# Feed-forward stage: the last block holds the last 384 tokens in their own order, and its output is stored by plain DMAs

## What is computed

```python
# q, k, v: (4, 8, 576, 64)
out_up    = repeat4(softmax(pool4(q) @ pool4(k).T / 8) @ pool4(v))
out_local = softmax(mask(|i-j| < 4, q @ k.T / 8)) @ v
x = (out_up + out_local).transpose(0, 2, 1, 3).reshape(2304, 512)
# experts: 8, each token goes to one
expert = argmax(normalise(x) @ normalise(emb).T / tau)
gate   = softmax(...)[expert]
x2[expert == e] = gate * (relu(x[expert == e] @ w1[e]) @ w2[e])   # 512 -> 1024 -> 512
# feed-forward: 512 -> 2048 -> 512
h   = x2 @ w_in
out = maximum(0.01 * h, h) @ w_out
```

## Time and profile before

| | us |
|---|---|
| median of 3 runs (lowest, highest) | 929.17 (929.08, 933.5) |
| profiled execution | 922.41 |
| its span | 920.6 |
| TensorE busy in the span | 873.1 (95%) |
| VectorE busy | 537.6 (58%) |
| ScalarE busy | 508.8 (55%) |
| GpSimd busy | 184.0 (20%) |

### The profile page before, as it was taken

The page is one execution under the profiler, slowest core; times in us unless marked ns, Lnnn a source line. Parts: engine busy times, 40 slices in busy tenths (PEclk is TensorE's granted clock), DMA queues, the critical chain, the costliest instruction groups (busy, mean ns, idle before and its releaser), DMA issues.

```text
span 920.6 us, 17203 instructions
## 1 busy us (share of the span) xinstructions
PE 873.1 (95%) x5878; PEld 733.8 (80%) x5878; DVE 537.6 (58%) x789; ACT 508.8 (55%) x912; POOL 184.0 (20%) x265
## 2 busy tenths in 40 slices
PE   8898997899999999999998999999999999999993
PEld 4787773677787777777777998998998998998992
DVE  5677766788888988888886543223223223223221
ACT  3677875788887888888885443223223223223221
POOL 8666773042510110120001002002002002001001
PEclk9999999999999999999999999999999999999997
DMA  7587567354727725541101002002002002000000
GB/s 221 163 236 205 182 223 256 111 192 131 289 53 278 275 94 238 224 144 47 35 23 46 1 1 69 1 1 69 0 0 68 0 0 68 0 0 35 1 1 34
DMA packets 44764, 92.39 MB, mean 100 GB/s; under 512 B 4712, under 2 KB 24040, under 8 KB 40624
## 3 DMA queue, kind: packets, MB, share of 16 engines
q1 hardware_dynamic: 34496, 43.48, 15.7%
q0 software_dynamic: 10224, 48.33, 14.1%
HBM read 72.98 MB, written 18.81 MB: 100 GB/s over the span
## 4 chain that ended last, share of the span: by engine, by line
PE 79%; DVE 6%; ACT 5%; issue 4%; POOL 2%; DMA 1%; SPq 1%; DVEq 0%; ACTq 0%; POOLq 0%
PE banks L857 68%; PE banks L795 2%; PE banks L889 2%; ACT ehi L1107 1%; PE banks L773 1%; PE banks L700 1%; DVE elo L1438 1%; DVE xTlo L1443 1%; PE banks L737 1%; PE banks L749 1%; PE banks L908 1%; PE banks L708 1%; PE banks L864 1%; PE banks L767 1%; ACT pdin L1010 1%
## 5 line engine op out<-in xcount | busy, mean ns | idle before, releaser
L1438 DVE TENSOR_TENSOR elo<-wslot,ehi 128x1024 fp32r<-128x1024 f32 x196 | 237.6, 1224 | 37.9 <-ACT ehi L1107 28.9
L1107 ACT ACTIVATE ehi<-wslot 128x1024 fp32r x196 | 204.9, 1059 | 45.4 <-PE banks L857 36.0
L1512 DVE SCALAR_TENSOR_TENSOR fg<-fraw 128x384 f32<-128x384 f32 x96 | 53.5, 558 | 212.3 <-ACT fraw L1194 212.3
L1194 ACT ACTIVATE fraw<-banks 128x384 f32<-128x384 f32 x96 | 47.2, 492 | 227.8 <-PE banks L857 227.5
L857 PE MATMUL banks<-zhi,winhi 128*128 (+1 forms) x384 | 130.5, 340 | 0.2 <-issue 0.2
L857 PE MATMUL banks<-zhi,winlo 128*128 (+1 forms) x384 | 129.4, 337 | 0.0
L857 PE MATMUL banks<-zlo,winhi 128*128 (+1 forms) x384 | 129.0, 336 | 0.0
L857 PE MATMUL banks<-wouthi,fhi 128*128 128x512 f32 x288 | 113.1, 393 | 3.5 <-DVE flo L1517 3.4
L857 PE MATMUL banks<-wouthi,flo 128*128 128x512 f32 x288 | 113.9, 395 | 0.0
L857 PE MATMUL banks<-woutlo,fhi 128*128 128x512 f32 x288 | 113.7, 395 | 0.0
L656 POOL DMA_INDIRECT out_x<-o_sb,row_tok x18 | 17.9, 995 | 386.0 <-ACT o_sb L1221 382.4
(11 more groups left out here) (206 smaller groups left out, 1432.2 us busy)
## 6 DMA issues: line engine op xcount, KB each, us to landing
wslot<-in_w POOLq DMA_DIRECT2D x24, 1024.0 KB, 9.4
wslot<-in_w SPq DMA_DIRECT2D x8, 1024.0 KB, 6.1
xr<-xs SPq DMA_DIRECT2D x25, 272.0 KB, 2.9
ys<-y_sb SPq DMA_DIRECT2D x25, 256.0 KB, 2.0
qb<-in_qT SPq DMA_DIRECT2D x16, 288.0 KB, 4.0
kb<-in_kT SPq DMA_DIRECT2D x16, 288.0 KB, 5.0
vq<-in_vtok SPq DMA_DIRECT2D x32, 144.0 KB
vwin<-in_vtok SPq DMA_DIRECT2D x16, 245.0 KB
```

The lines of the kernel that those rows point to most:

```text
L1107: act.activation(ehi[:, ring_at(k), :], wslot[:, chunk_cols(offs[dt], matrix, half, c)], ACT.Copy).then_inc(s_ehi, 1)
L1194: act.activation(fraw[:, f % 2, :], banks[:, f % 2, 0:TB], ACT.Copy).then_inc(s_fhev, 1)
L1438: dve.tensor_tensor(elo[:, ring_at(k), :], wslot[:, chunk_cols(offs[dt], matrix, half, c)], ehi[:, ring_at(k), :].bitcast(F32), ALU.subtra ...
L1512: dve.scalar_tensor_tensor(out=fg[:, f % 2, :], in0=fraw[:, f % 2, :], scalar=0.01, in1=fraw[:, f % 2, :], op0=ALU.mult, op1=ALU.max).then ...
```

## The change

Only the first 1920 rows in the order of the experts are built from the first 15 token tiles (`NSORT` = 15); tokens 1920 to 2303 stay in their own order and are block 5.

- `ranks` and `place` of the last batch also give `early`, the counts of the first 15 tiles alone. `LASTB` is 2, since two of the last batch's five tiles are among the first 15. In `place` of the last batch the running counts are updated after `pos`, not before it.
- `rank_at` and the gates' table are made for 15 tiles; for the last three, `rank_at[:, 0]` is worked out from `pos` directly, and their gates are written to `row_gate` by VectorE.
- The gates' scatters are 15 in place of 18, and `row_tok` has 15 columns.
- `gather(blk)` waits for three tiles of `ys` more.
- GpSimd scatters the output of blocks 0 to 4 alone. SyncE stores block 5's three output tiles by plain DMAs, each as soon as it is evicted, and waits for them.

```diff
@@ build @@
-    gates = nc.dram_tensor("gates", (N, 2), F32).ap()
+    gates = nc.dram_tensor("gates", (N - TB, 2), F32).ap()
...
+        EARLY = banks[:, 2, C_AT + E:C_AT + 2 * E]
...
+        NSORT = NTOK - TT
+        LASTB = (NB - 1) * TT - TILES[B - 1][0]
@@ SyncE, behind the last store_y @@
+            last = out[N - TB:N, :].rearrange("(t p) n -> p t n", p=P)
+            for i in range(TT):
+                sp.wait_ge(s_oev, TT * NB + i + 1)
+                sp.dma_start(last[:, i, :], o_sb[:, i, :]).then_inc(s_last, 16)
+            sp.wait_ge(s_last, 16 * TT)
@@ GpSimd @@
                 if e == SLOTS:
-                    put_gates(0, NTOK // 2)
+                    put_gates(0, NSORT // 2)
                 if e == SLOTS + 1:
-                    put_gates(NTOK // 2, NTOK)
+                    put_gates(NSORT // 2, NSORT)
...
-            gp.tensor_copy(row_tok[:], row_gate[:, :, 1]).then_inc(s_row_tok, 1)
+            gp.tensor_copy(row_tok[:, 0:NSORT], row_gate[:, 0:NSORT, 1]).then_inc(s_row_tok, 1)
...
             def gather(blk):
-                ready = min(NT, TT * (blk + 1) + E - 1)
+                ready = min(NT, TT * (blk + 2) + E - 1) if blk < NB - 1 else NT
...
-                scatter_out(blk)
-            gp.wait_ge(s_out, 16 * TT * NB)
+                if blk < NB - 1:
+                    scatter_out(blk)
+            gp.wait_ge(s_out, 16 * TT * (NB - 1))
@@ TensorE, ranks @@
+                if b == B - 1:
+                    for j in range(LASTB):
+                        m = pe.matmul(EARLY, onesb[:], ohb[:, j, :], start=(j == 0), stop=(j == LASTB - 1))
                 m.then_inc(s_rank, 1)
@@ VectorE, place @@
-                link(dve.tensor_tensor(run[:], COUNT, run[:], ALU.add))
+                if b < B - 1:
+                    link(dve.tensor_tensor(run[:], COUNT, run[:], ALU.add))
                 dve.tensor_reduce(pos[:, t0:t1], c, AX, ALU.add).then_inc(s_pos, 1)
+                if b == B - 1:
+                    link(dve.tensor_tensor(early[:], EARLY, run[:], ALU.add))
+                    link(dve.tensor_tensor(run[:], COUNT, run[:], ALU.add))
@@ VectorE, behind the tile table; the lines from the first reached to rank_at are the old ones, with early for cnt and columns a @@
+            link(dve.tensor_tensor(early[:], early[:], ebase[:], ALU.subtract))
+            dve.tensor_scalar(pad[:, 1, :], early[:], -1.0, float(REG), ALU.mult, ALU.add)
+            dve.tensor_scalar(pad[:, 2, :], ntile[:], float(P), float(-REG), ALU.mult, ALU.add)
+            dve.scalar_tensor_tensor(out=pad[:, 0, :], in0=ntile[:], scalar=float(P), in1=early[:],
+                                     op0=ALU.mult, op1=ALU.subtract)
+            link(dve.tensor_tensor_scan(sorted_end[:], ones_r[:], early[:], 0.0, ALU.mult, ALU.add))
+            sh, a = [NQ, NSORT, E - 1], slice(0, NSORT)
...
+            sh, z = [NQ, TT, E - 1], slice(NSORT, NTOK)
+            link(dve.tensor_tensor(region[:, z], reached[:, z], row(pad[0:NQ, 2, 0:E - 1], sh, 1), ALU.mult))
+            link(dve.tensor_reduce(rank_at[:, 0, z], region[:, z], AX, ALU.add))
+            link(dve.tensor_tensor(rank_at[:, 0, z], pos[:, z], rank_at[:, 0, z], ALU.add))
+            dve.tensor_copy(rank_i[:, 0, :], rank_at[:, 0, :])
+            dve.tensor_copy(rank_i[:, 1, a], rank_at[:, 1, a]).then_inc(s_rank_at, 1)
...
+            dve.reciprocal(row_gate[:, NSORT:NTOK, 0], gt1[:, NSORT:NTOK])
             dve.reciprocal(tok_gate[:, :, 0], gt1[:]).then_inc(s_tok_gate, 1)
```

More of the change, by code:

```diff
@@ L211, in build @@
         yg = sb("yg", [NQ, TB // NQ, DM])
+        early = sb("early", [P, E])
         riota_i = sb("riota_i", [NQ, NTOK], I32)
@@ L214, in build @@
         sorted_end = sb("sorted_end", [P, E])
-        pad = sb("pad", [P, 2, E])
+        pad = sb("pad", [P, 3, E])
         reached = sb("reached", [NQ, NTOK, E - 1])
@@ L324, in build @@
         s_out = sem("s_out")
+        s_last = sem("s_last")
         order = [(0, 0), (0, 1), (1, 0)]
@@ L628, in _ @@
                 if e == SLOTS:
[L629 removed]
+                    put_gates(0, NSORT // 2)
                 if e == SLOTS + 1:
[L631 removed]
+                    put_gates(NSORT // 2, NSORT)
                 if e == SLOTS + 2:
[L633 to L634 removed]
+                    gp.wait_ge(s_gput, 16 * NSORT)
+                    gp.dma_start(row_gate[:, 0:NSORT, :], gates.rearrange("(t p) c -> p t c", p=NQ)).then_inc(s_gget, 16)
                 gp.wait_ge(s_wl[e % SLOTS], 64 * (e // SLOTS))
@@ L1407, in _ @@
             dve.tensor_tensor(gt2[:], gt2[:], gt1[:].unsqueeze(2).broadcast_to(be), ALU.subtract).then_inc(s_gate, 1)
-            sh = [NQ, NTOK, E - 1]
[L1410 to L1417, removed]
-            link(dve.tensor_tensor(reached[:], row(pos[:], sh, 2), row(ebase[0:NQ, 1:E], sh, 1), ALU.is_ge))
@@ new lines, in _ @@
+            dve.tensor_scalar(pad[:, 2, :], ntile[:], float(P), float(-REG), ALU.mult, ALU.add)
[3 more added lines that the diff above has]
+            sh, a = [NQ, NSORT, E - 1], slice(0, NSORT)
+            link(dve.tensor_tensor(reached[:, a], row(riota[:, a], sh, 2), row(sorted_end[0:NQ, 0:E - 1], sh, 1), ALU.is_ge))
@@ new lines, in _ @@
+            link(dve.tensor_tensor(region[:, a], reached[:, a], row(pad[0:NQ, 0, 0:E - 1], sh, 1), ALU.mult))
+            link(dve.tensor_reduce(rank_at[:, 0, a], region[:, a], AX, ALU.add))
+            link(dve.tensor_tensor(rank_at[:, 0, a], riota[:, a], rank_at[:, 0, a], ALU.add))
+            sh = [NQ, NTOK, E - 1]
+            link(dve.tensor_tensor(reached[:], row(pos[:], sh, 2), row(ebase[0:NQ, 1:E], sh, 1), ALU.is_ge))
+            sh = [NQ, NSORT, E - 1]
+            link(dve.tensor_tensor(region[:, a], reached[:, a], row(pad[0:NQ, 1, 0:E - 1], sh, 1), ALU.mult))
@@ new lines, in _ @@
+            link(dve.tensor_reduce(rank_at[:, 1, a], region[:, a], AX, ALU.add))
+            link(dve.tensor_tensor(rank_at[:, 1, a], pos[:, a], rank_at[:, 1, a], ALU.subtract))
+            sh, z = [NQ, TT, E - 1], slice(NSORT, NTOK)
+            link(dve.tensor_tensor(region[:, z], reached[:, z], row(pad[0:NQ, 2, 0:E - 1], sh, 1), ALU.mult))
+            link(dve.tensor_reduce(rank_at[:, 0, z], region[:, z], AX, ALU.add))
+            link(dve.tensor_tensor(rank_at[:, 0, z], pos[:, z], rank_at[:, 0, z], ALU.add))
```

## The result

The changed kernel took 920.91 us (median of 4; 920.19 to 923.11), the kernel before beside it on the same chip 929.12 us (4 runs; 928.02 to 933.5). The ratio is 0.9908 (0.9887 to 0.993): faster, by 929.12 x 0.0092 = 8.5 us (the two medians alone lie 8.2 us apart). Forecast were 919.6 us and 9.6 us less; the time lies in the range.

The account below looks back on a forecast made before the run. TensorE's products, 79% of the 920.6 us span, can't shrink; what can go is the end, 7.9 us of it GpSimd's DRAIN. End 9.5 us and routing 0.14 off 929.17 gave 919.6 us, range 917.5 to 923.0.

Parts of the forecast that it names:

- The end: After VectorE's last eviction: SyncE's plain stores replace GpSimd's indirect ones, hiding GpSimd's 7.9 us DRAIN; 9.5 us saved, 8.4 to 9.6.
- A: Program's end: the 7.9 us belong to any program with such DMAs and come back behind SyncE's stores; 927.3 us, chance 0.07.
- B: Program's end: SyncE's DRAIN becomes the long one after waiting for its stores, 7.9 us for 0.13; 927.4 us, chance 0.03.
- The landing by the page: Block 5's plain stores: the skill page gives 2.3 us from issue to landing, where the trace row says 2.0.
- The routing's work: VectorE, behind the last positions: added counts, rank operations and reciprocal delay the first weight remainder by 1.3 us, to 160.2.
- The 0.14 us of earlier positions: Last batch's ranks: 0.20 us less on VectorE, 0.06 more on TensorE, so the last positions come 0.14 us earlier.
- The routing's cover: Before the first expert tile: VectorE's 1.47 us idle before the remainder of x hides the 1.3 us; cost 0, bound +1.0.
- case C: Rival: routing makes tile 0 1.0 us late and stores land in 3.1 us; 921.7 us, chance counted within the forecast's 0.86.
- The second cover: After tile 0's products: TensorE's 0.9 us wait for the next tile's rows from DRAM absorbs a late start of tile 0.
- Rival D: Before TensorE's first product: longer idle lowers its clock; slower only if 14.2 us are lost, two tiles give 945.4; chance 0.02.
- From span to median: Whole kernel: the gap between 922.41 us profiled and 929.17 median stays, so 9.6 us comes off the median.
- GpSimd's middle: GpSimd between routing and end: three fewer gate scatters and later gathers gain and cost 0, bound -1 for a weight stall.

## Why the prediction was right

**The end** was the gain, and for the reason given. Forecast 9.5 us (8.4 to 9.6), measured 9.7, just above the bound: 8.2 for the hidden DRAIN, 1.5 for issue and landing. Landing was the 2.0 us of the earlier trace rows. Of the 0.2 missed, 0.12 is SyncE's DRAIN, 13 ns where the sum had 130.

**Rivals A and B** fell at the first profile after. A (the tail belongs to the program): GpSimd's DRAIN runs once, at 852.8, and nothing of its kind follows the stores. The run in which GpSimd only waits shows what A left possible to be untrue as well: no outstanding transfer made it long. B (SyncE's DRAIN becomes long): 13 ns behind a wait for its stores. The Trainium skill (VectorE: DVE Perf Modes, The DRAIN you can't avoid) has the boilerplate DRAINs at some 12 ns on all five engines; SyncE's 13 ns agrees, GpSimd's 7829 to 8156 ns in every profile here does not. (The other engines' DRAINs are also longer, 0.7 to 2.4 us, but begin while the engine's last operation still runs and end with it: ScalarE's takes 717 ns from 913.6 on, its eviction 0.69 us from 913.57 on.)

**The landing by the page.** The Trainium skill (DMA: Bandwidth & Descriptors, latency and other measured facts) led to an estimate of 2.3 us for the plain store; the trace says 2.0 in all three, as the row of the expert stores had it.

**The routing's work** was priced right. Positions to first weight remainder: 158.91 - 147.44 = 11.47 us before, 160.24 - 147.38 = 12.86 after, +1.39. The forecast had 1.32 + 0.14 = 1.46, and the start at 160.2, where it came. Where the stage was long it was 168.76 - 155.63 = 13.13 us against the same 11.47 (167.22 - 155.75), +1.66. The 0.14 us of earlier positions are read from the first rank product, 147.44 - 146.32 = 1.12 us before and 155.63 - 154.68 = 0.95 in the changed kernel, 0.17 earlier:

```profile
154.68 0.18 PE L817 MATMUL banks<-ohb,tri 128*128 128x40 bf16 x1 [2.02 <-DVE ohb L1348]
```

**The routing's cover** is the weak step, and its size was off: "Cost taken: 0, bound +1.0". The cover, 1.47 us of VectorE's idle, was read from a profile in which the last scatter landed late. Where it lands late, nothing is lost: the idle left was 0.77 and 0.89 us, TensorE's first product waited its usual 1.41, and it came 5.3 us behind the issue of the first xr load in both kernels (163.48 - 158.16; changed 164.12 - 158.80). On the chips with the long stage the first xr load follows the positions sooner, 8.8 us (164.38 - 155.63; before 164.57 - 155.75) in place of 11.4. There the idle is gone in two of the three profiles of the changed kernel without added copies, and the remainder of x starts 15.4 us behind the positions in place of 14.4 (170.12 - 155.75): 1.0 us. The third, with the overlapped end, still has an idle, because TensorE ran at a granted clock of 0.60 from 164 to 168 us and turned x later:

```profile
171.55 0.69 DVE L1483 TENSOR_TENSOR xTlo<-banks,xThi 128x512 fp32r<-128x512 f32 x1 [0.88 <-ACT xThi L1131]
```

The pair with moved weights shows the loss on a chip with the short stage, 1.4 us. So case C's "1.0 us late" is what these rows show, without its slow landing. The second cover, the 0.9 us wait for the next tile's rows, stands in five profiles (0.7 to 1.0 us), all of them with a late landing, and so where it isn't needed.

**Rival D** was right as a mechanism and small in size. The wait before the first product did lengthen (in the unedited changed kernel 1.94 and 3.32 us in two of three profiles), and behind the longer one the clock fell and about 3 us went. It is far from the 14.2 us from which it would have decided.

**The median.** 8.5 us less, 9.6 forecast. The first measurement had the long stage, where the routing costs 1.0 us up to the first product, and 9.7 - 1.0 = 8.7. This fits, but isn't shown: the interval of the ratio is 6.5 to 10.5 us, and the chip of the short stage gave the same ratio. The two profiles with the long stage even speak against it: from the positions to the last block's first eviction the changed kernel took 757.9 us and the kernel before 757.7, so of the 1.0 us only 0.3 was left at the end, and the spans differ by 9.6. What gave the rest back isn't known; it is no more than profiles of one kernel differ by.

**From span to median.** "I keep the difference", 922.41 profiled and 929.17 in the median, turned out harmless but for no reason that the forecast gave. The profile of before was of the short kind, and its 922.41 us lie below every run of that kernel in the measurement (lowest 928.02). Another profile of the same kernel, on a chip where it takes 929 us as well, showed the long stage. So the difference lay in the attention stage, which the change leaves alone, and stayed.

**GpSimd's middle** cost nothing, as forecast: from first product to the last block's eviction 742.6 us in the kernel before, 741.8 and 742.6 in the changed one.

**What stays open.** What makes the attention stage 8 us longer on some chips. The trace names the waits only as coming from elsewhere. Less DMA in it did nothing on a chip where it was short; that was not tried where it is long. Open too is what GpSimd's DRAIN does in its 8 us.

## What to carry to other kernels

Read the list of each engine's last instructions: if one engine ends with a long fixed instruction, let its list end early and give the last work to an engine whose end is short. Before taking an idle as cover, ask what makes it long in this profile, and what it would be if that landing came sooner. Compare two profiles by stage and from landmark to landmark; here the spans differed by 2.2 us and the ends by 9.7.

## What the runs showed of the hardware

- GpSimd's DRAIN took 7829 to 8156 ns, with its last transfer just landed or some 65 us old; SyncE's 13 ns with its stores landed, 128 or 129 ns right behind an issue. The length of GpSimd's belongs to the program: it was the same to the nanosecond in all profiles of a kernel, on whatever chip (7911 in three of the kernel before, 8156 in three of the changed one and in the edited forms of it whose list issues the same transfers), and another where GpSimd's list issues others (7829, 7992, 8074).
- Expert 1's weights in flight delay the landing of the last scatter: on one chip the load behind it was issued 11.4 us after the positions with them and 8.8 in three profiles without. Over all profiles with the short stage and the weights in place it was 9.8 to 12.0.
- TensorE's clock after an idle: behind 2.90, 2.93, 3.31 and 3.32 us the granted clock was 0.50 to 0.60 in the mean of 4 us soon after, and 0.57 behind 2.00 and 2.02 us as well; behind 1.94, 1.97 and 2.34 us the products ran at full clock. Behind another 2.02 us, at 154.68 in the changed kernel, it was 1.00. The length of the idle alone doesn't decide it. The clearest rows are four profiles of the changed kernel and its edited forms, all with the long stage. In each TensorE runs the same 16 products of zeros, which keep it busy, idles 3.18 us, and runs 28 more of the kind. Granted clock 0.65 and 0.92 in 160 to 164 and 164 to 168 us in the first; 1.00 and 1.00 in the second (unedited, on another chip); 0.55 and 0.60 in the third; 0.77 and 0.50 in the fourth:

```profile
161.78 7.62 PE L683 MATMUL banks<-zrow 128*128 128x512 bf16 x28 [3.18 <-issue]
162.22 6.22 PE L683 MATMUL banks<-zrow 128*128 128x512 bf16 x28 [3.18 <-issue]
161.35 9.09 PE L685 MATMUL banks<-zrow 128*128 128x512 bf16 x28 [3.18 <-issue]
163.32 9.00 PE L683 MATMUL banks<-zrow 128*128 128x512 bf16 x28 [3.18 <-issue]
```

- The same program has a stage of two lengths, 8 us apart. On the three chips with more than one profile on record all profiles of a chip had the same one (four short, four short, three long).
